# Attention and two MoE layers on one core: the general path as a loop over query tiles, one factor worked out on the row, the last output tiles in another order

## The chip, the cores and the metric

The kernel runs on one core of a Trainium2 chip. The metric is the device time of one execution in microseconds (us). TensorE is called PE here, its weight loads PEld, VectorE DVE, ScalarE ACT, GpSimd POOL and SyncE SP. A letter q behind an engine's name (PEldq, DVEq, SPq) is its sequencer, which runs branches, waits and the issue of DMAs.

## The reference

Local attention with a few global keys and a distance bias, then a layer with SiLU and a layer with hard-swish, in float32.

```python
# q, k, v: (2, 8, 768, 64); n_global = 8, n_local = 96
scores = q @ k.transpose(0, 1, 3, 2) / 8
rel = pos[:, None] - pos[None, :]
keep = (pos[None, :] < n_global) | ((rel >= 0) & (rel < n_local))
dist = where(is_global & ~is_local, n_local, abs(rel))
a = softmax(where(keep, scores - slope[h] * dist, -1e9))
x = (a @ v) as (1536, 512)
h = x @ moe_w_in;   x = (h * sigmoid(h)) @ moe_w_out            # 512 -> 2048 -> 512
h = x @ moe2_w_in;  y = (h * clip(h + 3, 0, 6) / 6) @ moe2_w_out
```

## The kernel before

The program is written by hand: one block of code for each engine, with semaphores between them. `either` (L205) reads a flag that DVE works out from the two counts and branches on every engine: `banded` when at most 32 global keys and at most 97 local ones are asked for, else `general`. With 8 and 96, `banded` runs. In each engine's stream of instructions the code stands in this order: what is ahead of `either`, the banded body, a jump over the general body, the general body, what follows. On PE the jump is written at L209, and the general body that it skips has `2 * 6 * (2 + 6 + 6)` = 168 matmuls of the attention loop and the 42 of one step of `product`, each with its weight load.

The attention has 48 units (8 pairs of heads, 6 query tiles of 128). What follows are 4 blocks of 8 steps: two halves of the tokens through the first layer, two through the second. A step `s` multiplies by 256 columns of `w_in` in the seven products of a Strassen scheme (`product`, P1, P2, P6, P5, P7, P3, P4 in this order, 6 matmuls of 384 columns each), applies the gate, and multiplies by `w_out` (`down`), one step late. Every matmul is done in three float32r passes (`hi*hi`, `hi*lo`, `lo*hi`), so each weight and activation is split: ACT writes the `_hi` copies (`w_high`, `g_high`, `wo_high`), DVE the `_lo` parts (`w_low`, `g_low`), POOL the sums of `w_in` that the scheme needs (`w_sum`, four for each step) and `wo_low`.

The order around the end of the attention is written out by hand. PE finishes the banded body with all products of step 0 and the last `values`, jumps, and begins step 1. There P1 waits for `g_ok` (the last gate product of step 0, DVE L480), P5 for `c_ok` (the first `c_sum` of step 1, DVE L470), and P7 for the second `kept` of the step, which is ACT's copy `u_c`:

```python
elif n == P7:
    pe.wait_ge(kept, 3 * s + 2)
```

ACT's queue has in step 1 `keep(s, p1_c, 0, P1)`, then `w_high(2, 0)`, then `keep(s, u2_c, 0, P6)`. `w_high(2, 0)` waits for the four sums of step 2, which POOL makes in order after `wo_low(0)`, and `wo_low(0)` waits for the same `g_ok`. DVE's queue has `g_low(0, 0)`, `c_sum(1, 0)`, `g_low(0, 1)`, `w_low(2, 0)`.

At the end, PE does the last `down2` tile by tile (6 matmuls of 512 columns each), ACT copies tiles 0, 2 and 4 from PSUM, DVE tiles 1, 3 and, in two halves, 5, and SP stores each.

Of the kernel before, what the change touches and what calls it, by code (L numbers as in the profile page):

```python
# [12 lines left out]
P = 128  # L13
# [8 lines left out]
GLOB = 32  # L22
# [29 lines left out]


def at_least(eng, sem, value):

    if isinstance(value, int) and value <= 0:
        return
    eng.wait_ge(sem, value)


def build(nc, qT, kT, v, w_in1, w_out1, w_in2, w_out2, counts, out):
    outer = ExitStack()
    with outer:
# [18 lines left out]
        words = sb("words", [1, 4], I32)  # L82
        cnt = sb("cnt", [1, 8])
        ones = sb("ones", [1, P])
# [7 lines left out]
        with attn:  # L92
# [19 lines left out]
            with ExitStack() as general:  # L112

                a_tmp = [sb(f"a_tmp{i}", [P, S], F32, general) for i in range(7)]
                a_rel = sb("a_rel", [P, S], F32, general)
                a_far = sb("a_far", [P, S], F32, general)
# [55 lines left out]
        a_max = sem("a_max"); a_exp = sem("a_exp"); a_norm = sem("a_norm"); a_pt = sem("a_pt")  # L172
        a_prt_ok = sem("a_prt_ok"); a_pv = sem("a_pv"); a_x = sem("a_x")

# [42 lines left out]
        def _(sp):  # L217
# [32 lines left out]
            for s in range(2, NSTEP):  # L250
# [6 lines left out]
            for t in range(NT - 1):  # L257
                store(1, t)
            for a in range(2):
                sp.wait_ge(y_dve, HALF * 3 + HALF + a)  # L260
                sp.dma_start(out[1, NT - 1][:, QC * a:QC * a + QC], y_out[:, NT - 1, QC * a:QC * a + QC]).then_inc(stored, 16)
            sp.wait_ge(stored, 16 * (2 * NT + 1))

        @block.gpsimd
        def _(pool):
# [94 lines left out]
            def general():  # L360

                pool.wait_ge(k_in[1], NQK)
                pool.wait_ge(q_in[1], NQK)
                nc.gpsimd.iota(a_rel[:, :], [[-1, S]], base=0, channel_multiplier=1, **io).then_inc(iota_ok, 1)
                nc.gpsimd.iota(a_tmp[1][:, :], [[1, S]], base=0, channel_multiplier=0, **io).then_inc(iota_ok, 1)
# [22 lines left out]
        def _(dve):  # L388
            links = [0]

            def link(ins):

                links[0] += 1
                ins.then_inc(chain, 1)
                dve.wait_ge(chain, links[0])


            for h in range(2 * NH):
# [15 lines left out]
            nc.vector.tensor_scalar(cnt[:, 6:7], cnt[:, 5:6], 0.0, None, ALU.max).then_inc(row_ok, 1)  # L414
            link(nc.vector.tensor_scalar(cnt[:, 7:8], cnt[:, 5:6], 1.0, None, ALU.is_ge))
            link(nc.vector.scalar_tensor_tensor(cnt[:, 7:8], cnt[:, 5:6], float(MAXLOC), cnt[:, 7:8], ALU.is_le, ALU.mult))
            nc.vector.scalar_tensor_tensor(flag[:, :], cnt[:, 4:5], float(GLOB), cnt[:, 7:8], ALU.is_le,
                                           ALU.mult).then_inc(flag_ok, 1)
# [113 lines left out]
            def general():  # L532
                rel, jj, loc, glb, keep, ngl, dist = [a[:, :] for a in a_tmp]
                halves = lambda ap: ap.rearrange("p (a k) -> p a k", a=2)
# [7 lines left out]
                dve.sem_inc(a_score, 1)  # L542
                NLINK = 126

                with dve.Fori(0, NPAIR) as it:
                    count = [0]

                    def link(ins):

                        count[0] += 1  # L550
                        ins.then_inc(a_link, 1)
                        dve.wait_ge(a_link, NLINK * it + count[0] + 1)


                    for t in range(NT):
                        link(nc.vector.tensor_scalar(rel, a_rel[:, :], float(P * t), None, ALU.add))
                        masks(link, rel, jj, loc, glb, keep, ngl, dist)
                        link(nc.vector.tensor_scalar(a_far[:, :], keep, -MASKED, MASKED, ALU.mult, ALU.add))
                        for h in range(2):
# [15 lines left out]
                            nc.vector.tensor_scalar(a_pr[:, :], a_pr[:, :], a_one[:, 4:5], None, ALU.mult).then_inc(a_norm, 1)  # L575

                    assert count[0] == NLINK, count[0]
                for s in range(2):
# [80 lines left out]
            for a in range(2):  # L659
                nc.vector.tensor_copy(y_out[:, NT - 1, QC * a:QC * a + QC], y_bank(NT - 1)[:, QC * a:QC * a + QC]).then_inc(y_dve, 1)  # L660

        @block.scalar
        def _(act):
# [110 lines left out]
            def general():  # L774
                act.sem_inc(a_x, 1)
                with act.Fori(0, NPAIR) as it:
                    for t in range(NT):
                        for h in range(2):
# [7 lines left out]
                        act.wait_ge(a_pv, 2 * NT * it + 2 * t + 2)  # L786
                        nc.scalar.activation(x_raw[:, bass.ds(it, 1), P * t:P * t + P].rearrange("p a t -> p (a t)"),
                                             ps[:, 4, 0:P], ACT.Copy).then_inc(a_x, 1)
# [70 lines left out]
            act.wait_ge(stored, 16 * NT)  # L859
            for t in (0, 2, 4):  # L860
                act.wait_ge(y_tile, t + 1)
                nc.scalar.activation(y_out[:, t, :], y_bank(t), ACT.Copy).then_inc(y_act, 1)

        @block.tensor
        def _(pe):
# [104 lines left out]
            def general():  # L970
                with pe.Fori(0, NPAIR) as it:
                    for t in range(NT):
                        for h in range(2):
                            step = 2 * NT * it + 2 * t + h + 1
                            if t == 0 and h == 0:
                                pe.wait_ge(k_in[0], NQK * (it + 1))
                                pe.wait_ge(q_in[0], NQK * (it + 1))
                                pe.wait_ge(v_in[0], 16 * (it + 1))
                            pe.wait_ge(a_score, step)
                            for b in range(2):  # L980
# [32 lines left out]

            def down2(s, c, t):

                for n, (wo, g) in enumerate(((wo_hi, g_hi), (wo_lo, g_hi), (wo_hi, g_lo))):
                    mm = nc.tensor.matmul(y_bank(t), g[:, s % 2, c, P * t:P * t + P], wo[:, s % 2, DM * c:DM * c + DM],  # L1017
                                          start=s % STEPS == 0 and c == 0 and n == 0,
                                          stop=s % STEPS == STEPS - 1 and c == 1 and n == 2)
                return mm  # L1020
# [35 lines left out]
            pe.wait_ge(g_lo_ok, 2 * s + 2)  # L1056
            for t in range(NT):
                down2(s, 0, t)
                down2(s, 1, t).then_inc(y_tile, 1)

# [44 lines left out]
```

## Time and profile before

| | us |
|---|---|
| median of 3 runs | 605.09 |
| lowest, highest | 604.94, 606.37 |
| profiled execution | 604.28 |
| its span | 602.2 |

| engine | busy us | share of the span |
|---|---|---|
| PE | 591.2 | 98% |
| PEld | 515.6 | 86% |
| DVE | 374.9 | 62% |
| ACT | 341.3 | 57% |
| POOL | 285.1 | 47% |

The span is the time from the first to the last instruction of the core; 2.1 us of the profiled execution's time lie around it. Busy PE counts pipelined matmuls with modelled ends, so 98% means that matmuls follow each other nearly everywhere. What counts is where they don't, and what each of these gaps waits for.

### The profile page before, as it was taken

How to read it: one execution, taken by the hardware profiler on the slowest of the kernel's cores; microseconds unless marked ns; L12 is line 12 of the kernel's file. 1: busy time of each engine (PE TensorE's matmuls, PEld its weight loads, DVE VectorE, ACT ScalarE, POOL GpSimd, SP SyncE). 2: the span in 40 equal slices, each digit the busy share in tenths (PEclk: the TensorE clock that was granted, in tenths of full speed). 3: DMA queues.
4: the chain of work that ended last, by engine and by line, in shares of the span. 5: the costliest groups of instructions: out<-in, count | busy, mean ns of one | idle time of the engine just before them, and what ended most of it. 6: DMA issues, size and time to landing. Idle time of an engine off the chain costs nothing.

```text
span 602.2 us, 9602 instructions
## 1 busy us (share of the span) xinstructions
PE 591.2 (98%) x3423; PEld 515.6 (86%) x3423; DVE 374.9 (62%) x697; ACT 341.3 (57%) x658; POOL 285.1 (47%) x353
## 2 busy tenths in 40 slices
PE   7999998999999999999999999999999999999997
PEld 4665557999999999999999998999999989999996
DVE  6678985766755568557555966575556685555331
ACT  6789886445454467444444665544457565555441
POOL 4787994757933314439433234395333343331110
PEclk9999999899999999999999999999999999999999
DMA  8434430132222112211222123113221252220002
GB/s 355 152 116 169 151 119 4 36 140 72 70 71 71 71 35 89 85 53 56 71 70 71 36 70 106 70 36 101 72 69 41 70 175 70 71 71 35 1 0 106
DMA packets 14597, 50.08 MB, mean 83 GB/s; under 512 B 1618, under 2 KB 1874, under 8 KB 14546
## 3 DMA queue, kind: packets, MB, share of 16 engines
q1 hardware_dynamic: 14258, 48.63, 23.5%
q10 hardware_dynamic: 288, 0.79, 0.4%
q8 instruction: 29, 0.48, 0.3%
q14 instruction: 22, 0.18, 0.1%
HBM read 46.27 MB, written 3.15 MB: 82 GB/s over the span
## 4 chain that ended last, share of the span: by engine, by line
PE 88%; POOL 6%; issue 2%; ACT 2%; DVE 2%; DVEq 0%; DMA 0%; ACTq 0%
PE ps L941 38%; PE ps L1017 22%; PE ps L1008 15%; PE ps L1009 8%; POOL probs L283 3%; PE ps L888 2%; PE ps L898 2%; PE ps L913 2%; POOL rsume L275 1%; ACT probs L673 1%; POOL x_t L323 0%; POOL x_t L320 0%; POOL x_t L315 0%; DVE x_lo L464 0%; DVE g_f L480 0%
## 5 line engine op out<-in xcount | busy, mean ns | idle before, releaser
L328 POOL TENSOR_TENSOR wo_lo<-wo_raw,wo_hi 128x1024 fp32r<-128x1024 f32 x32 | 77.3, 2416 | 258.8 <-ACT wo_hi L741 251.4
L941 PE MATMUL ps<-x_hi,wi_hi 128*128 128x384 f32 x448 | 151.5, 338 | 2.3 <-issue 2.3
L941 PE MATMUL ps<-x_lo,wi_hi 128*128 128x384 f32 x448 | 150.7, 336 | 0.0
L941 PE MATMUL ps<-x_hi,wi_lo 128*128 128x384 f32 x448 | 150.5, 336 | 0.0
L470 DVE TENSOR_TENSOR c_sb<-ps,p_c 128x384 f32<-128x384 f32 x64 | 35.6, 557 | 159.3 <-PE ps L941 159.3
L721 ACT ACTIVATE p_c<-ps 128x384 f32<-128x384 f32 x64 | 31.5, 492 | 126.4 <-PE ps L941 126.0
L941 PEld LDWEIGHTS ps<-x_hi,wi_hi 128*128 128x128 f32 x448 | 84.6, 189 | 5.5 <-issue 2.8
L941 PEld LDWEIGHTS ps<-x_hi,wi_lo 128*128 128x128 f32 x448 | 84.6, 189 | 0.5
L941 PEld LDWEIGHTS ps<-x_lo,wi_hi 128*128 128x128 f32 x448 | 84.6, 189 | 0.0
L1017 PE MATMUL ps<-wo_hi,g_lo 128*128 128x512 f32 x192 | 75.0, 391 | 0.0
L1017 PE MATMUL ps<-wo_lo,g_hi 128*128 128x512 f32 x192 | 75.0, 390 | 0.0
L1017 PE MATMUL ps<-wo_hi,g_hi 128*128 128x512 f32 x192 | 74.7, 389 | 0.0
L809 ACT ACTIVATE g_hi<-g_f 128x768 fp32r<-128x768 f32 x64 | 50.6, 839 | 42.4 <-DVE g_f L480 25.3
L455 DVE TENSOR_TENSOR wi_lo<-wi_raw,wi_hi 128x896 fp32r<-128x896 f32 x64 | 71.9, 1157 | 0.2 <-ACT wi_hi L702 0.2
L702 ACT ACTIVATE wi_hi<-wi_raw 128x896 fp32r<-128x896 f32 x64 | 57.4, 938 | 2.3 <-POOL wi_raw L300 2.3
L1008 PE MATMUL ps<-g_hi,wo_lo 128*128 128x512 f32 x128 | 50.0, 391 | 0.0
L1008 PE MATMUL ps<-g_lo,wo_hi 128*128 128x512 f32 x128 | 50.0, 391 | 0.0
L1008 PE MATMUL ps<-g_hi,wo_hi 128*128 128x512 f32 x128 | 50.0, 391 | 0.0
L673 ACT ACTIVATE probs<-negs,negmax 128x256 f32<-128x256 f32 (+1 forms) x96 | 45.9, 480 | 6.2 <-DVE negmax L491 5.8
L283 POOL TENSOR_SCALAR probs<-probs,rinv 128x256 f32<-128x256 f32 (+1 forms) x96 | 45.2, 484 | 4.1
L491 DVE CUSTOM_DVE_ANT_0 negs<-ps,m_bias 128x256 f32<-128x256 f32 (+1 forms) x96 | 37.3, 391 | 15.8 <-PE ps L888 12.6
L1017 PEld LDWEIGHTS ps<-wo_hi,g_lo 128*128 128x128 f32 x192 | 36.0, 188 | 7.5
(95 smaller groups left out, 1095.1 us busy)
## 6 DMA issues: line engine op xcount, KB each, us to landing
wi_raw<-in_w_in SPq DMA_DIRECT2D x32, 512.0 KB, 3.4
wo_raw<-in_w_out SPq DMA_DIRECT2D x32, 512.0 KB, 3.4
v_raw<-in_v SPq DMA_DIRECT2D x8, 704.0 KB, 4.2
k_raw<-in_kT SPq DMA_DIRECT2D x8, 464.0 KB, 4.9
out_y<-y_out SPq DMA_DIRECT2D x11, 256.0 KB, 4.5
q_raw<-in_qT SPq DMA_DIRECT2D x6, 384.0 KB, 5.8
q_raw<-in_qT ACTq DMA_DIRECT2D x2, 384.0 KB, 4.0
out_y<-y_out SPq DMA_DIRECT2D x2, 128.0 KB, 1.8
```

The source lines that it names most:

```text
L283: nc.gpsimd.tensor_scalar(probs[:, u % DEEP, h, a:256], probs[:, u % DEEP, h, a:256], rinv[:, u % DEEP, h:h + 1], 1.0, ALU.mult, ALU.mult) ...
L328: nc.gpsimd.tensor_tensor(wo_lo[:, s % 2, :], wo_raw[:, s % 2, :], wo_hi[:, s % 2, :], ALU.subtract).then_inc(wo_lo_ok, 1)
L455: nc.vector.tensor_tensor(wi_lo[:, s % 2, at], wi_raw[:, s % 2, QC + 7 * P * part:QC + 7 * P * part + 7 * P], wi_hi[:, s % 2, at], ALU.sub ...
L470: nc.vector.tensor_tensor(c_sb[:, i, :], p_bank(bank), add[:, :], ALU.add).then_inc(c_ok, 1)
L491: nc.vector.tensor_tensor_reduce(negs[:, u % 2, h, 0 if t else P:256], sc, bi, -0.125, 3.0e38, ALU.add, ALU.min, negmax[:, u % DEEP, h:h + ...
L673: nc.scalar.activation(probs[:, u % DEEP, h, a:256], negs[:, u % 2, h, a:256], ACT.Exp, bias=negmax[:, u % DEEP, h:h + 1], scale=-1.0, acc ...
L702: nc.scalar.activation(wi_hi[:, s % 2, at], wi_raw[:, s % 2, QC + 7 * P * part:QC + 7 * P * part + 7 * P], ACT.Copy).then_inc(wi_hi_ok, 1)
L809: nc.scalar.activation(g_hi[:, s % 2, f, :], g_f[:, f, :, :].rearrange("p a t -> p (a t)"), ACT.Copy, scale=1.0 if s < NSTEP // 2 else 1.0 ...
L941: mm = nc.tensor.matmul(p_bank(bank), w[:, s % 2, at], x[:, b, k, :], start=fresh and k == 0 and i == 0, stop=k == 1 and i == 2, skip_grou ...
L1008: nc.tensor.matmul(y_bank(i), wo[:, s % 2, w], g[:, s % 2, c, 0:512], start=first, stop=last)
L1009: mm = nc.tensor.matmul(y_bank(4 + i // 2)[:, 256 * (i % 2):256 * (i % 2) + 256], wo[:, s % 2, w], g[:, s % 2, c, 512:S], start=first and ...
L1017: mm = nc.tensor.matmul(y_bank(t), g[:, s % 2, c, P * t:P * t + P], wo[:, s % 2, DM * c:DM * c + DM], start=s % STEPS == 0 and c == 0 and ...
```

## The change

The general path, which does not run with these inputs, becomes a loop over the query tiles inside the loop over pairs, on PE, DVE and ACT. On the path that runs, DVE works out `-8 * n_local` on the one-row tile `cnt` before the flag, where `base` did it later on 128 partitions; the broadcast matmul carries four columns for three, and waits for two semaphore steps. The last `down2` goes by the table `LAST`: tiles 0 to 3, the first half of tile 4, tile 5, the second half of tile 4.

```diff
+LAST = ((0, 0, slice(0, DM)), (1, 1, slice(0, DM)), (2, 2, slice(0, DM)), (3, 3, slice(0, DM)),
+        (4, 4, slice(0, QC)), (5, 5, slice(0, DM)), (6, 4, slice(QC, DM)))
+LAST_DVE = (1, 3, 6)
...
+            for i, t, cols in LAST:
+                dve_before = sum(j < i for j in LAST_DVE)
+                if i in LAST_DVE:
+                    sp.wait_ge(y_dve, HALF * 3 + dve_before + 1)
+                else:
+                    sp.wait_ge(y_act, HALF * 3 + i - dve_before + 1)
+                sp.dma_start(out[1, t][:, cols], y_out[:, t, cols]).then_inc(stored, 16)
...
             nc.vector.tensor_scalar(cnt[:, 6:7], cnt[:, 5:6], 0.0, None, ALU.max).then_inc(row_ok, 1)
+            nc.vector.tensor_scalar(cnt[:, 7:8], cnt[:, 5:6], -8.0, 0.0, ALU.mult, ALU.min).then_inc(row_ok, 1)
...
-                link(nc.vector.tensor_copy(nums[:, 0:3], ps[:, 1, 0:3]))
+                link(nc.vector.tensor_copy(nums[:, :], ps[:, 1, 0:4]))
...
-                link(nc.vector.tensor_scalar(nums[:, 3:4], nl, -8.0, None, ALU.mult))
...
-            for t in (1, 3):
-                dve.wait_ge(y_tile, t + 1)
-                nc.vector.tensor_copy(y_out[:, t, :], y_bank(t)).then_inc(y_dve, 1)
-            dve.wait_ge(y_tile, NT)
-            for a in range(2):
-                nc.vector.tensor_copy(y_out[:, NT - 1, QC * a:QC * a + QC], y_bank(NT - 1)[:, QC * a:QC * a + QC]).then_inc(y_dve, 1)
+            for i, t, cols in LAST:
+                if i in LAST_DVE:
+                    dve.wait_ge(y_tile, i + 1)
+                    nc.vector.tensor_copy(y_out[:, t, cols], y_bank(t)[:, cols]).then_inc(y_dve, 1)
...
-            pe.wait_ge(row_ok, 1)
-            nc.tensor.matmul(ps[:, 1, 0:3], ones[:, :], cnt[:, 4:7], start=True, stop=True).then_inc(rows_ok, 1)
+            pe.wait_ge(row_ok, 2)
+            nc.tensor.matmul(ps[:, 1, 0:4], ones[:, :], cnt[:, 4:8], start=True, stop=True).then_inc(rows_ok, 1)
...
                 with pe.Fori(0, NPAIR) as it:
-                    for t in range(NT):
+                    with pe.Fori(0, NT) as t:
                         for h in range(2):
...
-                                                      q_raw0[D * h:D * h + D, P * t:P * t + P],
+                                                      a_q[D * h:D * h + D, :],
...
-            for t in range(NT):
-                down2(s, 0, t)
-                down2(s, 1, t).then_inc(y_tile, 1)
+            for i, t, cols in LAST:
+                if cols.start:
+
+                    pe.wait_ge(y_act, HALF * 3 + 3)
+                down2(s, 0, t, cols)
+                down2(s, 1, t, cols).then_inc(y_tile, 1)
```

Three places in the order of instructions. The first is PE, from the last `values` of the banded body through the jump (L209) into the general body; `a_pr` and `a_prT` are that body's probabilities. Before:

```order
L913 MATMUL ps<-probsT,v_raw 64x128 x4
L209 UNCONDITIONAL_BRANCH
L971 UNCONDITIONAL_BRANCH
L971 ISA
L979 ISA
L981 MATMUL ps<-k_raw,q_raw 128x384 x2
L988 MATMUL ps<-ident,a_pr 128x128 x6
L992 ISA
L995 MATMUL ps<-a_prT,v_raw 64x128 x6
L979 REGISTER_ALU
```

and of the change, at the same place:

```order
L926 MATMUL ps<-probsT,v_raw 64x128 x4
L215 UNCONDITIONAL_BRANCH
L984 UNCONDITIONAL_BRANCH
L985 UNCONDITIONAL_BRANCH
L985 ISA
L991 ISA
L993 ISA
L995 MATMUL ps<-k_raw,a_q 128x384 x2
L1002 MATMUL ps<-ident,a_pr 128x128 x6
L1009 MATMUL ps<-a_prT,v_raw 64x128 x6
L991 REGISTER_ALU
```

The group of 2, 6 and 6 matmuls stands 12 times before and twice in the change, 168 and 28 matmuls; the 42 of `product` follow in both. The jump at the head leads past all of it.

The second is DVE ahead of and behind the branch of `either`, up to the first wide operation of `base`. Before:

```order
L414 TENSOR_SCALAR cnt<-cnt 1x1
L415 TENSOR_SCALAR cnt<-cnt 1x1
L416 SCALAR_TENSOR_TENSOR cnt<-cnt 1x1
L417 SCALAR_TENSOR_TENSOR flag<-cnt 1x1
L208 TENSOR_LOAD flag
L208 ISA x2
L209 COMPARE_AND_BRANCH
L424 COPY nums<-ps 128x3
L440 TENSOR_SCALAR nums<-nums 128x1
L442 TENSOR_SCALAR x_t<-x_t,nums 128x384
```

and of the change:

```order
L422 TENSOR_SCALAR cnt<-cnt 1x1
L423 TENSOR_SCALAR cnt<-cnt 1x1
L424 TENSOR_SCALAR cnt<-cnt 1x1
L425 SCALAR_TENSOR_TENSOR cnt<-cnt 1x1
L426 SCALAR_TENSOR_TENSOR flag<-cnt 1x1
L214 TENSOR_LOAD flag
L214 ISA x2
L215 COMPARE_AND_BRANCH
L433 COPY nums<-ps 128x4
L450 TENSOR_SCALAR x_t<-x_t,nums 128x384
```

One operation on a single element is added ahead of the flag, and the one at L440 is gone behind the branch.

The third is SP's queue at the end of the program, the last weights and the stores of the second half of the tokens. Before:

```order
L194 DMA wi_raw<-in_w_in 128x1024
L199 DMA wo_raw<-in_w_out 128x1024 x2
L248 DMA out_y<-y_out 128x512 x5
L261 DMA out_y<-y_out 128x256 x2
L63 UNCONDITIONAL_BRANCH
```

and of the change:

```order
L200 DMA wi_raw<-in_w_in 128x1024
L205 DMA wo_raw<-in_w_out 128x1024 x2
L269 DMA out_y<-y_out 128x512 x4
L269 DMA out_y<-y_out 128x256
L269 DMA out_y<-y_out 128x512
L269 DMA out_y<-y_out 128x256
L68 UNCONDITIONAL_BRANCH
```

A whole tile now stands between the two halves, and the halves are of tile 4.

## Rows read from the trace of the kernel before

**Rows 1.** The page, part 1: busy time of each engine.

```profile
PE 591.2 (98%) x3423; PEld 515.6 (86%) x3423; DVE 374.9 (62%) x697; ACT 341.3 (57%) x658; POOL 285.1 (47%) x353
```

**Rows 2.** The page, part 4: the chain that ended last, by line.

```profile
PE ps L941 38%; PE ps L1017 22%; PE ps L1008 15%; PE ps L1009 8%; POOL probs L283 3%; PE ps L888 2%; PE ps L898 2%; PE ps L913 2%; POOL rsume L275 1%; ACT probs L673 1%; POOL x_t L323 0%; POOL x_t L320 0%; POOL x_t L315 0%; DVE x_lo L464 0%; DVE g_f L480 0%
```

**Rows 3.** Line 209 by engine: count, duration min/median/max in ns, first and last start.

```profile
L209 ACTq COMPARE_BRANCH  x2: 43/44/45, 3.8 to 103.5; - x2
L209 PEldq COMPARE_BRANCH  x2: 78/2039/4000, 3.9 to 101.5; - x2
L209 DVEq COMPARE_BRANCH  x2: 50/56/63, 4.0 to 97.7; - x2
```

**Rows 4.** The same chain in order of time: start us, us, what.

```profile
102.97 1.04 DVE g_f L480 x2
104.01 1.69 issue
105.70 9.16 PE ps L941 x42
114.86 0.23 PE ps L1008
115.09 0.12 PE ps L1009
...
123.19 7.28 PE ps L941 x42
```

**Rows 5.** Stretches: length, busy PE, PEld, DVE, ACT, POOL, granted clock, DMA share, GB/s.

```profile
103.44:105.70 2.26, 0.00 (x1) 0.03 (x1) 1.44 (x3) 2.03 (x3) 1.62 (x1) 1.00 0.01 4
...
106.55:109.97 3.42, 3.42 (x13) 3.42 (x12) 1.45 (x3) 0.49 (x1) 3.34 (x4) 0.50 0.47 153
110.00:114.70 4.70, 4.70 (x28) 4.62 (x27) 3.58 (x5) 3.01 (x6) 4.62 (x6) 1.00 0.00 0
```

**Rows 6.** POOL in order of time after 104 us: start us, us, what [idle before].

```profile
104.08 2.36 POOL L328 TENSOR_TENSOR wo_lo<-wo_raw,wo_hi 128x1024 fp32r<-128x1024 f32 x1 [7.36 <-DVE g_f L480]
106.40 1.45 POOL L292 TENSOR_TENSOR wi_raw<-wi_raw 128x256 f32<-128x256 f32 x1
...
109.30 0.73 POOL L300 TENSOR_TENSOR wi_raw<-wi_raw 128x256 f32<-128x256 f32 x1
109.99 1.46 POOL L292 TENSOR_TENSOR wi_raw<-wi_raw 128x256 f32<-128x256 f32 x1
```

**Rows 7.** ACT in order of time after 107 us.

```profile
107.30 0.49 ACT L721 ACTIVATE p_c<-ps 128x384 f32<-128x384 f32 x1 [1.78 <-PE ps L941]
110.07 0.96 ACT L702 ACTIVATE wi_hi<-wi_raw 128x896 fp32r<-128x896 f32 x1 [2.27 <-POOL wi_raw L300]
110.93 0.47 ACT L721 ACTIVATE u_c<-ps 128x384 f32<-128x384 f32 x1
```

**Rows 8.** DVE in order of time after 104 us.

```profile
104.82 2.44 DVE L598 TENSOR_TENSOR g_lo<-g_f,g_hi 128x768 fp32r<-128x768 f32 x1 [0.82 <-ACT g_hi L809]
109.22 0.56 DVE L470 TENSOR_TENSOR c_sb<-ps,p_c 128x384 f32<-128x384 f32 x1 [1.97 <-PE ps L941]
109.70 1.15 DVE L598 TENSOR_TENSOR g_lo<-g_f,g_hi 128x768 fp32r<-128x768 f32 x1
```

**Rows 9.** PE in order of time: the 25th matmul of step 1, P7's first.

```profile
111.53 0.36 PE L941 MATMUL ps<-x_hi,wi_hi 128*128 128x384 f32 x1
```

**Rows 10.** The chain at the start of the program.

```profile
2.61 0.07 DVE cnt L415
...
4.26 0.16 DVE nums L440
4.43 0.03 issue
```

**Rows 11.** The end: DVE and SP in order of time, and one stretch.

```profile
599.14 0.76 DVE L660 COPY y_out<-ps 128x256 f32<-128x256 f32 x2 [2.03 <-PE ps L1017]
599.59 0.81 SPq L261 DMA_DIRECT2D out_y<-y_out  x2
...
600.40:601.40 1.00, 0.00 (x0) 0.00 (x0) 0.00 (x0) 0.00 (x0) 0.00 (x0) 1.00 0.78 262
```

More of the change, by code:

```diff
@@ L112, in build @@
             with ExitStack() as general:
-                a_tmp = [sb(f"a_tmp{i}", [P, S], F32, general) for i in range(7)]
+                a_tmp = [sb(f"a_tmp{i}", [P, S], F32, general) for i in range(6)]
                 a_rel = sb("a_rel", [P, S], F32, general)
+                a_q = sb("a_q", [P, P], F32, general)
                 a_far = sb("a_far", [P, S], F32, general)
@@ L256, in _ @@
                         store(0, t)
-            for t in range(NT - 1):
-                store(1, t)
-            for a in range(2):
-                sp.wait_ge(y_dve, HALF * 3 + HALF + a)
-                sp.dma_start(out[1, NT - 1][:, QC * a:QC * a + QC], y_out[:, NT - 1, QC * a:QC * a + QC]).then_inc(stored, 16)
-            sp.wait_ge(stored, 16 * (2 * NT + 1))
+            for i, t, cols in LAST:
[5 more added lines that the diff above has]
+                sp.dma_start(out[1, t][:, cols], y_out[:, t, cols]).then_inc(stored, 16)
+            sp.wait_ge(stored, 16 * (NT + len(LAST)))
         @block.gpsimd
@@ L414, in _ @@
             nc.vector.tensor_scalar(cnt[:, 6:7], cnt[:, 5:6], 0.0, None, ALU.max).then_inc(row_ok, 1)
[L415 to L417 removed]
+            nc.vector.tensor_scalar(cnt[:, 7:8], cnt[:, 5:6], -8.0, 0.0, ALU.mult, ALU.min).then_inc(row_ok, 1)
+            link(nc.vector.tensor_scalar(cnt[:, 8:9], cnt[:, 5:6], 1.0, None, ALU.is_ge))
+            link(nc.vector.scalar_tensor_tensor(cnt[:, 8:9], cnt[:, 5:6], float(MAXLOC), cnt[:, 8:9], ALU.is_le, ALU.mult))
+            nc.vector.scalar_tensor_tensor(flag[:, :], cnt[:, 4:5], float(GLOB), cnt[:, 8:9], ALU.is_le,
                                            ALU.mult).then_inc(flag_ok, 1)
@@ L532, in general @@
             def general():
-                rel, jj, loc, glb, keep, ngl, dist = [a[:, :] for a in a_tmp]
+                jj, loc, glb, keep, ngl, dist = [a[:, :] for a in a_tmp]
                 halves = lambda ap: ap.rearrange("p (a k) -> p a k", a=2)
@@ L542, in general, with link @@
                 dve.sem_inc(a_score, 1)
-                NLINK = 126
+                NLINK = 22
                 with dve.Fori(0, NPAIR) as it:
[L546 to L552, printed above, removed]
-                    for t in range(NT):
-                        link(nc.vector.tensor_scalar(rel, a_rel[:, :], float(P * t), None, ALU.add))
-                        masks(link, rel, jj, loc, glb, keep, ngl, dist)
+                    with dve.Fori(0, NT) as t:
+                        count = [0]
+                        def link(ins):
+                            count[0] += 1
+                            ins.then_inc(a_link, 1)
+                            dve.wait_ge(a_link, (NLINK * NT + 1) * it + NLINK * t + count[0] + 1)
+                        masks(link, a_rel[:, :], jj, loc, glb, keep, ngl, dist)
                         link(nc.vector.tensor_scalar(a_far[:, :], keep, -MASKED, MASKED, ALU.mult, ALU.add))
@@ L775, in general @@
                 act.sem_inc(a_x, 1)
+                x_tiles = x_raw[:, :, :].rearrange("p n (t k) -> p (n t) k", k=P)
                 with act.Fori(0, NPAIR) as it:
-                    for t in range(NT):
+                    with act.Fori(0, NT) as t:
+                        act.wait_ge(q_in[0], NQK * (it + 1))
+                        act.wait_ge(a_score, 2 * NT * it + 2 * t + 1)
+                        nc.scalar.activation(a_q[:, :], q_raw0[:, bass.ds(P * t, P)], ACT.Copy).then_inc(a_qt, 1)
                         for h in range(2):
@@ L859, in _ @@
             act.wait_ge(stored, 16 * NT)
-            for t in (0, 2, 4):
-                act.wait_ge(y_tile, t + 1)
-                nc.scalar.activation(y_out[:, t, :], y_bank(t), ACT.Copy).then_inc(y_act, 1)
+            for i, t, cols in LAST:
+                if i not in LAST_DVE:
+                    act.wait_ge(y_tile, i + 1)
+                    nc.scalar.activation(y_out[:, t, cols], y_bank(t)[:, cols], ACT.Copy).then_inc(y_act, 1)
         @block.tensor
@@ L1012, in down1, with down2 @@
                 return mm
-            def down2(s, c, t):
+            def down2(s, c, t, cols=slice(0, DM)):
                 for n, (wo, g) in enumerate(((wo_hi, g_hi), (wo_lo, g_hi), (wo_hi, g_lo))):
-                    mm = nc.tensor.matmul(y_bank(t), g[:, s % 2, c, P * t:P * t + P], wo[:, s % 2, DM * c:DM * c + DM],
-                                          start=s % STEPS == 0 and c == 0 and n == 0,
-                                          stop=s % STEPS == STEPS - 1 and c == 1 and n == 2)
+                    mm = nc.tensor.matmul(y_bank(t)[:, cols], g[:, s % 2, c, P * t:P * t + P],
+                                          wo[:, s % 2, DM * c + cols.start:DM * c + cols.stop], start=s % STEPS == 0 and c == 0 and n == 0,
+                                          stop=s % STEPS == STEPS - 1 and c == 1 and n == 2, skip_group_check=True)
                 return mm
@@ L1056, in _ @@
             pe.wait_ge(g_lo_ok, 2 * s + 2)
-            for t in range(NT):
-                down2(s, 0, t)
-                down2(s, 1, t).then_inc(y_tile, 1)
+            for i, t, cols in LAST:
+                if cols.start:
+                    pe.wait_ge(y_act, HALF * 3 + 3)
+                down2(s, 0, t, cols)
+                down2(s, 1, t, cols).then_inc(y_tile, 1)
 def kernel(q, k, v, n_global, n_local, moe_w_in, moe_w_out, moe2_w_in, moe2_w_out):
```

20 lines of the change are left out of this document (11 added, 9 removed).

## The prediction

> **What bounds the kernel now.** I read the page first. PE is busy in 98% of the span [rows 1], and the chain that ended last lies on PE's matmuls for most of its length [rows 2]. So the time moves by what lies between PE's matmuls, and most of the changed lines (the general path) never run. In order of time the chain shows one gap that no producer explains: DVE's last gate product ends at 104.01, then 1.69 us of "issue", then PE's 42 products of step 1 from 105.70 [rows 4]. The view of line 209 names it. PE's second branch instruction there, the jump past the general body, lasts 4000 ns from 101.5; the same jump takes 43 ns on ACT and 63 on DVE [rows 3]. PE is idle from 103.44 to 105.70, and the granted clock then falls to 0.50 (1.2 of 2.4 GHz) for 3.4 us from 106.55 [rows 5]. Therefore the 42 products take 9.16 us, where the same 42 of a later step take 7.28 [rows 4].
>
> **The jump.** The length of the skipped code is what differs. PE skips 168 + 42 matmuls with their weight loads, 420 instructions and some dozens of waits and register operations; DVE's jump passes 126 linked operations with a wait each and costs nothing. After the change PE skips 28 + 42 matmuls, 140 instructions and their waits, less than DVE does now. I take PE's jump then at DVE's 63 ns, with 4000 ns as the other end. The Trainium skill has a rule for it (Runtime: NRT & Kernel Launch, section Instruction fetch mechanics): a taken branch whose target lies outside the window of two pages of 256 instructions stalls for a fetch; by it PE's jump would miss before and hit after, the same two values.
>
> Without the stall PE's step 1 starts when P1's own wait for `g_ok` is over, at 104.01 plus the 0.05 or so of a handover, 104.08: 1.6 us earlier. The obvious sum is then 1.6 for the gap plus 9.16 - 7.28 = 1.9 for the clock, 3.5 us less. I don't believe it, because of what is due next.
>
> **Where the stall goes.** P7, the fifth product of the step, waits for ACT's `u_c`. ACT does `u_c` behind `w_high(2, 0)`, which has idled 2.27 us for POOL's fourth sum, and starts at 110.07; `u_c` lies from 110.93 to 111.40 [rows 7], and P7's first matmul starts at 111.53 [rows 9]. POOL's own sequence began at 104.08, released by the same DVE product as P1, and runs without a pause through `wo_low(0)` and four sums until 110.03 [rows 6]. Nothing in it depends on PE's jump. P7 can therefore not start before about 111.45, however early PE comes. Without stall and at full clock PE has done P1, P2, P6 and P5 (24 matmuls at 7.28 / 42 = 0.173, 4.2 us) at 108.3; P5 waits for `c_sum(1, 0)`, which waits for DVE's `g_low(0, 0)` until 107.26 [rows 8], so it rather ends at 109.1. PE then stands for 2.4 us or more before P7. The low clock of the present run fell just where there was this slack. So of 3.5 us nothing is left at P7.
>
> **And two costs come with it.** First, POOL and DVE hold each other up. POOL's sum takes 0.73 us alone, and 1.45 and 1.46 in the two places where it meets a `g_low` of DVE [rows 6, 8]; `g_low(0, 0)` itself takes 2.44 beside `wo_low(0)`, against 1.15 of the next one. Now `c_sum(1, 0)` and `g_low(0, 1)` come at 109.22 and 109.70, when the last sum of step 2 is under way, and hurt only a sum of step 3. In the change PE's P2 is done early, `c_sum(1, 0)` follows `g_low(0, 0)` at 107.26, and `g_low(0, 1)` at 107.8, in the middle of the sums of step 2: one of them costs 0.73 more, and `w_high`, `u_c` and P7 shift to about 112.2. Ends: 0, if POOL holds what they share each time, and 0.95, the whole of a `g_low`. The Trainium skill says why (SBUF — State Buffer, section Who interferes with whom): a VectorE operation with two SBUF inputs and a GpSimd operation that reads SBUF exclude each other for a whole instruction, whoever starts first. By that rule `c_sum`, which reads PSUM, does not collide, and the row of 109.22 beside the sum of 109.30 at 0.73 agrees; the delay would be the same 0.73 to 0.95.
>
> Second, the clock. PE idle for 2.26 us brought it down [rows 5]. In the change PE is idle for 0.6 us at 103.5, some 0.7 before P5 and 2.4 to 3.1 before P7, no less in sum and in one piece longer. I expect it to fall again, now after P7 has started or shortly before, where PE has no slack and the chain is matmuls alone. A low spell on the path costs 9.16 - 7.28 = 1.9 us; if it begins in the gap some of it is hidden. I take 1.6, with ends 0 and 1.9.
>
> **The small parts.** Start: the chain passes through L440, 0.19 us with its handover [rows 10], which goes; ahead of the flag one more operation on one element costs the 0.07 of L415 [rows 10], and the branch chain behind the flag shifts by it. Net -0.1; the fourth column of the small matmul is nothing beside these. End: the split of tile 4 replaces 6 matmuls of 0.23 by 12 of 0.12 (the two paces of the chain [rows 4]), +0.1. Behind the last matmul stand two copies, 0.76 us, and two issues [rows 11]; one copy and one issue stay, about -0.35. But tile 5's 256 KB is now issued only about half a us before the last 128 KB, and at the 262 GB/s of the stretch in which the final 256 KB went [rows 11] these two need 1.5 us in the queue, one behind the other. So about half of the gain is lost. End: -0.15, bounds -0.3 and +0.1. The wait for ACT's copy of the first half of tile 4 is covered by the 6 matmuls of tile 5 (1.4 us against a copy below 0.76). ACT's and DVE's own jumps cost nothing now and cannot gain.
>
> **Sum.** Against the profiled execution's 604.28: P7 later +0.7, low clock on the path +1.6, start -0.1, end -0.15, together +2.05, 606.3. The profiled execution is 0.8 below the median of the runs, 605.09; they spread over 1.4 us, and I read this as the low spell falling in other places of the same step, outside the slack that it found in the profiled one. On the median the sum gives 607.1. As the other runs already pay some of the clock, I forecast between the two, **606.8 us**, with 605.9 to 607.9 for this case.
>
> **Rivals.** (1) The gain is real: P7 is not held, because POOL's sums come earlier or `u_c` does. PE would be ahead by 1.6 us and, with a shorter idle, keep its clock: 604.3 - 3.5 - 0.25 = 600.5 to 603 on the side of faster. For it speaks only that the gap is the largest "issue" on the chain; against it ACT's 2.27 us of idle for POOL, and POOL's unbroken sequence. It decides if `u_c` ends before 109.8. 10%. (2) The stall goes, P7 waits, but the clock does not fall on the path (the idle pieces are short enough, or the spell lies in the gap): only the collision is left, 605.09 + 0.7 - 0.25 = 605.5, or 604.8 without it. For it speaks that PE's new idle is cut in three by P1 to P5; against it the 2.26 us in one piece that were enough, and the last piece is as long. 15%. (3) The jump is no cheaper: something other than the length of the skipped code makes PE's 4000 ns, its queue for one. Then only start and end are left, 604.8. The jump of DVE, also long, speaks mildly for it. 12%. The forecast itself has 60%; 3% is for the rest, such as other pieces of code that now lie across a fetch.
>
> **Range and chances.** What a measurement of this kernel can tell from no change is about 0.3%, 1.8 us. The forecast case is nearly half above 606.9, where slower begins, and half below; the rivals (2) and (3) are all within. Slower 0.36 with a little for a late clock in (2), within 0.3% 0.54, faster 0.10, which is rival (1). The range has to take in (2) and (3) and leaves out (1): 604.5 to 607.9.
>
> **What would show it.** In the profile of the changed kernel the branch at L215 on PE lasts under 0.1 us and step 1 starts at about 104 (if 4000 again: rival 3). P7's first matmul starts at 111.4 to 112.4 behind an idle of over 2 us put down to ACT's `u_c` (if at 108 to 110: rival 1). `g_low(0, 1)` starts before 108 and one of the sums of step 2 takes about 1.45. The granted clock is at 0.50 for some 3.4 us within 109 to 116. The last copy is one of 256 columns. The prediction is wrong above all if `u_c` is not what PE waits for next, or if the clock stays up.

## The result, and the profile after

Median of the changed kernel 608.98 us (606.38 to 610.46, 19 runs), of the kernel before on the same chip 606.24 (602.90 to 607.79, 19 runs): ratio 1.0050, 95% interval 1.0036 to 1.0064. It is slower, and 1.1 us above the upper end of the range predicted. The ratios here and below leave out runs in the slow state and are not the quotients of the two medians.

The forecast started from 605.09 us, the median of 3 runs of the kernel before. With 19 runs that median is 606.24, so 1.15 us of the distance to the forecast lie in this base. The change itself was forecast at +0.28% (606.8 for 605.09) and measured at +0.50%.

The profiled execution took 607.72 us, its span is 606.0 against 602.2. Part 1 of the page of the changed kernel answers to [rows 1]: six matmuls more, and PE busy for 3.5 us more.

```profile
PE 594.7 (98%) x3429; PEld 516.4 (85%) x3429; DVE 369.2 (61%) x696; ACT 341.6 (56%) x659; POOL 284.1 (47%) x353
```

Line 215 by engine (count, min/median/max in ns, first and last start) answers to [rows 3]. PE's jump past the general body is 310 ns for 4000:

```profile
L215 PEldq COMPARE_BRANCH  x2: 78/194/310, 4.0 to 100.0; - x2
L215 DVEq COMPARE_BRANCH  x2: 50/56/63, 4.0 to 96.3; - x2
```

The chain in order of time (start us, us, what) answers to [rows 4]. The "issue" of 1.69 is gone from behind the gate product; in its place the chain leaves PE and goes through POOL's four sums and ACT's `u_c` to P7:

```profile
101.50 1.04 DVE g_f L488 x2
102.61 2.40 POOL wo_lo L336
105.01 1.40 POOL wi_raw L300
106.42 1.41 POOL wi_raw L302
107.83 0.69 POOL wi_raw L305
108.58 0.73 POOL wi_raw L308
109.62 0.57 issue
110.20 0.48 ACT u_c L728
110.72 4.76 PE ps L954 x18
```

PE in order of time, the instructions that it idled ahead of (in brackets how long, and for whom): P1 follows at once, P5 waits 0.31, P7 waits 3.05 for ACT.

```profile
102.68 0.41 PE L954 MATMUL ps<-x_hi,wi_hi 128*128 128x384 f32 x1 [0.73 <-DVE g_f L488]
106.35 0.44 PE L954 MATMUL ps<-x_hi,wi_hi 128*128 128x384 f32 x1 [0.31 <-DVE c_sb L478]
110.72 0.69 PE L954 MATMUL ps<-x_hi,wi_hi 128*128 128x384 f32 x1 [3.05 <-ACT u_c L728]
```

Two stretches (start and end, then length, busy PE, PEld, DVE, ACT, POOL, granted clock, DMA share, GB/s) answer to [rows 5]: the idle piece, in which POOL is busy nearly throughout, and the spell at 0.50 that follows it, now partly on PE's own path:

```profile
107.66:110.72 3.06, 0.01 (x1) 0.00 (x1) 0.40 (x1) 1.38 (x3) 2.98 (x6) 0.94 0.02 7
110.32:113.74 3.42, 3.02 (x9) 3.02 (x10) 1.85 (x2) 1.24 (x4) 3.34 (x4) 0.50 0.00 0
```

DVE and POOL in order of time show the collision. `g_low(0, 1)` comes at 106.22, which is 3.7 us after the last gate product; in [rows 8] it is 5.7 us. The second sum of `w_in`, at 106.38, takes 1.44 for the 0.73 that it takes alone in [rows 6]:

```profile
105.75 0.55 DVE L478 TENSOR_TENSOR c_sb<-ps,p_c 128x384 f32<-128x384 f32 x1
106.22 1.02 DVE L607 TENSOR_TENSOR g_lo<-g_f,g_hi 128x768 fp32r<-128x768 f32 x1
106.38 1.44 POOL L302 TENSOR_TENSOR wi_raw<-wi_raw 128x256 f32<-128x256 f32 x1
```

So far it is what was forecast in kind. Counted from the end of the last gate product of step 0, step 2 starts after 21.13 us, in the kernel before after 19.03: +2.1. P7 starts 0.65 us later (8.19 for 7.54), and from there to step 2 it is 1.45 more, at the low clock. The prediction had 0.7 and 1.6 for these two, +2.3.

**Where the rest is.** The two spans differ by 3.8 us. The attention ended 1.5 us earlier in this execution; over the traces of this case the gate product ends anywhere from 102.5 to 105.8, so that is scatter. Step 1 gives +2.1, and from the start of step 2 to the end it is 482.33 us for 479.16, +3.2, where the prediction saw only the end of the program, at -0.15. The chain of the changed kernel shows a step of `down2` in the second layer and the last piece:

```profile
539.33 8.40 PE ps L1031 x36
...
586.43 16.83 PE ps L1031 x78
```

And the chain of the kernel before, for the same:

```profile
567.23 8.20 PE ps L1017 x36
...
582.74 16.38 PE ps L1017 x72
```

The same 36 matmuls take 8.40 for 8.20. One such step as a stretch, first of the changed kernel, then of the kernel before:

```profile
539.17:547.57 8.40, 8.40 (x38) 6.76 (x37) 6.15 (x8) 4.10 (x6) 0.93 (x1) 1.00 0.05 19
```

```profile
536.05:544.26 8.21, 8.21 (x38) 6.77 (x37) 6.16 (x8) 4.11 (x6) 0.94 (x1) 1.00 0.08 32
```

PE doesn't wait in either, the clock is 1.00 in both, and the other engines and the transfers do the same or less. Each `down2` matmul is 5.5 ns slower, 0.2333 us for 0.2278 from start to start (8.40 and 8.20 over 36), in all 16 steps of the second layer, 16 x 0.2 = 3.2 us. The products stay as they were, 7.30 us for 42 in both. A step of `down` in the first layer has 24 pairs, each a matmul of 512 and one of 256 columns; a pair takes 0.3472 for 0.3466, 0.015 us in a step and 0.2 in the layer. With 0.25 gained at the end this makes the +3.2. The diff as shown ahead of the prediction leaves out the one line that touches this:

```diff
-        cnt = sb("cnt", [1, 8])
+        cnt = sb("cnt", [1, 9])
```

SBUF is the memory in which the tiles stand. They are placed there one behind the other in steps of 32 bytes; no trace prints the places, so they are worked out here from the declared shapes. With nine words for eight everything allotted behind `cnt` stands 32 bytes further on. `g_hi` and `g_lo` are behind it, `wo_hi`, `wo_lo`, the `x` and the `wi` tiles ahead of it. A `down2` matmul reads one tile of each kind: it loads `g` as weights and streams `wo`.

### The profile page after: what moved, and what is told of

Read it like the earlier page. It is cut to its first block, busy times and chain, and to the rows that moved or that the text cites. A ratio compares the mean times of both kernels' runs of the same rounds, so it can differ in the third digit from the quotient of the medians.

```text
span 606.0 us, 9614 instructions
## 1 busy us (share of the span) xinstructions
PE 594.7 (98%) x3429; PEld 516.4 (85%) x3429; DVE 369.2 (61%) x696; ACT 341.6 (56%) x659; POOL 284.1 (47%) x353
## 4 chain that ended last, share of the span: by engine, by line
PE 88%; POOL 6%; ACT 2%; DVE 2%; issue 1%; DMA 0%; DVEq 0%; ACTq 0%
PE ps L954 38%; PE ps L1031 22%; PE ps L1022 14%; PE ps L1023 8%; POOL probs L291 3%; PE ps L926 2%; PE ps L911 2%; PE ps L901 2%; POOL rsume L283 1%; ACT probs L680 1%; POOL wo_lo L336 0%; POOL x_t L323 0%; POOL x_t L328 0%; DVE x_lo L472 0%; DVE g_f L488 0%
## 5 line engine op out<-in xcount | busy, mean ns | idle before, releaser
L1031 PE MATMUL ps<-wo_hi,g_lo 128*128 128x512 f32 (+1 forms) x194 | 76.3, 393 | 0.0
L1031 PE MATMUL ps<-wo_lo,g_hi 128*128 128x512 f32 (+1 forms) x194 | 76.3, 393 | 0.0
L1031 PE MATMUL ps<-wo_hi,g_hi 128*128 128x512 f32 (+1 forms) x194 | 76.2, 393 | 0.0
```

Of the source, the lines that this page charges most:

```text
L1031: mm = nc.tensor.matmul(y_bank(t)[:, cols], g[:, s % 2, c, P * t:P * t + P], wo[:, s % 2, DM * c + cols.start:DM * c + cols.stop], start=s ...
```

## The experiments

Theory A: the place of `g_hi` and `g_lo` costs the 3.2 us. Rival B: something in the code of the general path or in step 1 does. A third question is what the jump alone is worth, and a fourth, whether `u_c` is really all that PE waits for. The medians are of 5 to 12 runs, those of the kernel before of 17 to 33; each ratio is to runs of the kernel before on the same chip. The expectations give the old pace as 0.2272 us; over a whole step it is 0.2278.

**e1_before_cnt9**: the kernel before, with that one line.

```diff
-        cnt = sb("cnt", [1, 8])
+        cnt = sb("cnt", [1, 9])
```

> The kernel before with one edit: cnt has 9 words for 8, and every tile allotted behind it (g_hi, g_lo, y_out, the attention's tiles) lies 32 bytes further on. No instruction changes. Theory A (places in memory): the 36 matmuls of a down2 step take 8.39 us for 8.20 as in the changed kernel, 16 steps, so 3.0 us or 0.5% slower than before, with step 1 as before (jump of 4.0 us, P7 at once behind P5). Theory B (the pace of down2 comes from the changed code, or from the chip in that one execution): no difference from before, pace 0.2272 us.

608.49 against 604.98, ratio 1.0066 (1.0041 to 1.0091). From step 2 to the end 482.60, for 479.16. The chain has the slow step:

```profile
569.34 8.40 PE ps L1017 x36
```

One word more on a one-row tile makes the old program 0.4 to 0.9% slower. Its step 1 is also worth a look (PE in order of time): with the long jump the start of P1 is late, and P7 idles all the same.

```profile
103.73 0.41 PE L941 MATMUL ps<-x_hi,wi_hi 128*128 128x384 f32 x1 [1.73 <-issue]
110.76 0.44 PE L941 MATMUL ps<-x_hi,wi_hi 128*128 128x384 f32 x1 [2.59 <-ACT u_c L721]
```

Here the granted clock stays at 1.00, and step 2 starts 19.74 after the gate product; the expectation, that P7 follows P5 at once as in [rows 4], did not come true. The profiled execution of [rows 4] and [rows 5] had the low spell right behind the jump; in this one nothing held P2 back, so `c_sum` and `g_low(0, 1)` came early (106.11 and 106.59) and met the third sum, which took 1.44. The collision is thus no property of the change:

```profile
107.10 1.44 POOL L297 TENSOR_TENSOR wi_raw<-wi_raw 128x256 f32<-128x256 f32 x1
```

**e2_after_aligned**: the changed kernel with `cnt` as `[1, 17]`, which puts the tiles behind it 64 bytes from their old places. If what counts were 64-byte alignment, the pace would be back.

```diff
-        cnt = sb("cnt", [1, 9])
+        cnt = sb("cnt", [1, 17])
```

> The changed kernel with cnt of 17 words, so that all tiles behind it lie 64 bytes further on than before instead of 32. Theory A (places in memory): down2 goes back to 0.2272 us a matmul, about 3 us less than the changed kernel, and what is left against before is the 2.1 us of step 1 less 0.2 of start and end: 0.2 to 0.35% slower than before. Theory B (code or chance): as the changed kernel, 0.5% slower than before.

611.61 against 604.98, 1.0117 (1.0090 to 1.0144): slower still. `down2` keeps its slow pace, and now the first layer is slow too, 0.3528 for a pair (0.15 us more in each of its 16 steps). The chain, then one step of `down` as a stretch in e2 and in the kernel before:

```profile
574.40 8.40 PE ps L1031 x36
```

```profile
132.37:140.84 8.47, 8.47 (x50) 7.39 (x49) 6.57 (x8) 3.96 (x6) 1.31 (x2) 1.00 0.15 51
```

```profile
130.30:138.62 8.32, 8.32 (x49) 7.33 (x49) 7.88 (x7) 3.96 (x6) 6.57 (x5) 1.00 0.19 64
```

Alignment to 64 bytes is refuted; the place as such is not.

**e3_short_general**: the kernel before with the general path of the change alone, in the same tiles; start, `cnt` and the end of the program are the old ones.

```diff
-                    for t in range(NT):
+                    with pe.Fori(0, NT) as t:
...
-                                                      q_raw0[D * h:D * h + D, P * t:P * t + P],
+                                                      a_q[D * h:D * h + D, :],
```

> The kernel before with the general path of the changed one, and nothing else of the change (cnt of 8 words, the broadcast of 3 columns, the old last tiles). Theory A (the short jump moves the stall to P7 and the low clock behind it): PE's jump under 0.4 us, idle of 3 us before P7, 12.5 us for the 42 products of step 1 against 8.8 (first to last start), step 2 starts 2.1 us later counted from DVE's last gate product: 0.2 to 0.4% slower than before. Rival (the 0.5% comes from memory places alone and the step 1 loss is made up later): no difference from before.

606.70 against 604.98, 1.0025 (1.0006 to 1.0043). From step 2 to the end 479.18, the old pace. The jump is 310 ns, and step 1 looks as in the changed kernel, with a longer spell on the path (PE in order of time, then the stretch):

```profile
110.95 0.69 PE L953 MATMUL ps<-x_hi,wi_hi 128*128 128x384 f32 x1 [3.04 <-ACT u_c L728]
```

```profile
109.77:116.60 6.83, 5.65 (x18) 5.65 (x19) 3.26 (x5) 2.97 (x6) 5.74 (x5) 0.50 0.00 0
```

Step 2 starts 22.32 after the gate product, 1.2 later than expected. So B falls for what lies behind step 1, where the code of the general path costs nothing; and the jump that it shortens gives nothing.

**e4_uc_first**: e2's kernel with ACT's `w_high(2, 0)` moved behind the step's last `keep`, so that `u_c` needn't wait for POOL.

```diff
                 keep(s, p1_c, 0, P1)
-                if s == 1:
-                    w_high(2, 0)
...
                 keep(s, p5_c, 1, P5)
+                if s == 1:
+                    w_high(2, 0)
```

> The changed kernel with cnt of 17 words and, in step 1 alone, ACT's u_c and the next p_c ahead of w_high(2, 0). Theory A (P7 waits for u_c only because it is queued behind w_high): P7 follows P5 with at most 0.5 us of idle, the clock stays at 1.00, the 42 products take under 8.0 us, and step 2 starts 3.5 us or so earlier than in the changed kernel: 0.2 to 0.4% faster than before. Rival (another product of POOL or DVE holds P7 or P3 next): the idle of 2 to 3 us comes back at P3, P4 or down, and the time stays at or above that of before.

609.87 against 604.98, 1.0092 (1.0067 to 1.0118), 1.7 us under e2. The traces show 0.63 us of it in step 1; the intervals overlap, and the rest is not told from scatter. P7 starts without idle 4.97 us after the gate product, for 8.19. But two products later, at P4, PE waits again, now for DVE. The clock falls there too, to 0.50 in the microseconds 113 to 115:

```profile
112.42 0.69 PE L954 MATMUL ps<-x_hi,wi_hi 128*128 128x384 f32 x1 [2.42 <-DVE c_sb L478]
```

DVE in order of time shows what stands ahead of that `c_sum` in its queue, `w_low(2, 0)`, which waits for ACT's `w_high`:

```profile
110.59 1.30 DVE L463 TENSOR_TENSOR wi_lo<-wi_raw,wi_hi 128x896 fp32r<-128x896 f32 x1 [3.12 <-ACT wi_hi L709]
```

**e5_both_orders**: e3's kernel, with ACT's order of e4 and DVE's `w_low(2, 0)` behind both later `c_sum`s of the step.

```diff
                 if s == 1:
                     g_low(0, 1)
-                    w_low(2, 0)
...
                 c_sum(s, 2, 1, u2_c, P3)
+                if s == 1:
+                    w_low(2, 0)
```

> e3's kernel (the kernel before with the short general path, its tiles where they were) and, in step 1 alone, two orders changed: ACT's u_c and next p_c ahead of w_high(2, 0), and DVE's w_low(2, 0) behind c_sum(1, 1) and c_sum(1, 2). Theory A (P7 and then P4 wait only for what is queued behind the weights of step 2): no idle of PE over 0.8 us in step 1, clock at 1.00 through it, step 2 starts 16.4 us after DVE's last gate product of step 0 (19.0 before, 22.5 in e3's trace): 2.6 us or 0.4% faster than before. Rival (the gap is the sum of all that POOL has to do for step 2, and comes back in down or at step 2's P1): step 2 starts 18 us or more after that product, same time as before or slower.

602.55 against 606.45, 0.9943 (0.9921 to 0.9965). Step 2 starts 17.67 after the gate product (e3: 22.32; expected 16.4). PE in order of time has only short waits, the longest for the late `w_low`:

```profile
107.91 0.44 PE L954 MATMUL ps<-x_hi,wi_hi 128*128 128x384 f32 x1 [0.31 <-DVE c_sb L476]
121.76 0.44 PE L954 MATMUL ps<-x_hi,wi_hi 128*128 128x384 f32 x1 [1.08 <-DVE wi_lo L461]
```

and the clock stays up where it was at 0.50 in e3:

```profile
108.00:112.00 4.00, 4.00 (x23) 4.00 (x24) 1.98 (x4) 1.68 (x4) 3.92 (x5) 1.00 0.28 110
```

**e6_g_32, e7_g_128, e11_g_256, e8_all_32**: the kernel before with nothing but a tile of padding, 32, 128 or 256 bytes, ahead of `g_hi`; and with 32 bytes ahead of `x_raw`, which moves both operands of each matmul together.

```diff
+        sb("g_pad", [P, 8])            # e6; [P, 32] in e7, [P, 64] in e11
         g_hi = sb("g_hi", [P, 2, 2, 2 * TB], F32R)
```

```diff
+        sb("x_pad", [P, 8])            # e8
         x_raw = sb("x_raw", [P, NPAIR, S])
```

> The kernel before with 32 bytes left free ahead of g_hi: only g_hi, g_lo and y_out lie 32 bytes further on, everything else is where it was. Theory A (it is g's place, the weights of down2): down2 at 0.2332 us a matmul for 0.2272, down1 at 0.347, the products at 0.1735, 0.5% slower than before. Rival (it is another tile's place, of those that DVE, ACT and POOL work on): down2 stays at 0.2272.

> The kernel before with 128 bytes left free ahead of g_hi, so that g_hi and g_lo start at a multiple of 512 bytes (their 128-column blocks are 512 bytes long). Theory A1 (what counts is where a block of weights begins by itself, and whole 512 bytes are best): down2 at or under 0.2272 us. Theory A2 (what counts is the distance from wo's tiles, which is 0 mod 256 before and not now): down2 at 0.233 or above, down1 pairs at 0.353 as with a shift of 64.

> The kernel before with 32 bytes left free ahead of x_raw: all large tiles lie 32 bytes further on, their distances are as before. Theory A2 (distance between the two tiles that a matmul reads): all paces as before, 0.2272 and 0.1735, time the same. Theory A1 (the place itself): down2 at 0.233 and the products, whose weights move too, above 0.1735 as well; at 6 ns a matmul for all 2500 or so, over 10 us or 2% slower.

> The kernel before with 256 bytes left free ahead of g_hi. If what counts is the distance between the two tiles of a matmul modulo 256 bytes, down2 is at 0.2272 us and a down1 pair at 0.3466, time as before. If it is modulo 512 bytes or more, down2 is at 0.232 or above as with 32, 64 and 128.

| kernel | median, before | ratio (95%) | step 2 to end | 36 matmuls of `down2` |
|---|---|---|---|---|
| e6, g +32 | 608.42, 606.45 | 1.0029 (1.0008 to 1.0051) | 482.61 | 8.40 |
| e7, g +128 | 610.78, 606.45 | 1.0087 (1.0056 to 1.0117) | 483.65 | 8.37 |
| e11, g +256 | 605.16, 606.68 | 0.9983 (0.9959 to 1.0008) | 479.22 | 8.20 |
| e8, all +32 | 604.78, 606.45 | 0.9984 (0.9961 to 1.0006) | 479.20 | 8.20 |

The rows of the chain, of e6, e7, e8 and e11:

```profile
572.56 8.40 PE ps L1018 x36
```

```profile
572.35 8.37 PE ps L1018 x36
```

```profile
569.70 8.20 PE ps L1018 x36
```

```profile
568.74 8.20 PE ps L1018 x36
```

`g_hi` alone by 32 bytes is enough; all tiles together by 32 do nothing. What counts is where `g` stands relative to the tiles ahead of it. The candidate is the distance between the two tiles that a `down2` matmul reads, `g` and `wo`: no other pair is read together by the matmuls that slow down, and the products, which read neither, keep their pace. No run moved `wo` alone, so that it is this pair is argued and not shown. From the declared shapes `g_hi` - `wo_hi` is 63744 bytes, 249 x 256, in the kernel before. 256 more keeps the pace, 32, 64 and 128 more lose it. e7 refutes that any multiple of 128 will do.

These four also have the long jump, and their step 1 shows how it varies with it: P7 idles for over 2 us in e6, e7 and e8, its start is 8.17 to 8.18 after the gate product, and step 2 starts after 19.75, 21.39, 21.44 and, in e11, 19.03. PE's jump is itself not always as long; of line 210, e7 and e11:

```profile
L210 PEldq COMPARE_BRANCH  x2: 87/1704/3320, 3.9 to 100.3; - x2
L210 PEldq COMPARE_BRANCH  x2: 78/1939/3800, 3.9 to 103.0; - x2
```

Of the six traces with the long jump, the two with the longest (4.0 us in the kernel before, 3.8 in e11) have PE idle for 2.26 and 2.10 us ahead of P1, a low spell right behind it, no wait at P7 and the earliest step 2, 19.03. In the other four the jump takes 3.3 to 3.6, PE idles 1.59 to 1.81 ahead of P1, the clock stays up there, and P7 waits. In e7 and e8 the clock fell behind P7's idle, on the path (e8, PE in order of time, and a stretch):

```profile
112.19 0.45 PE L942 MATMUL ps<-x_hi,wi_hi 128*128 128x384 f32 x1 [2.54 <-ACT u_c L722]
```

```profile
113.18:116.60 3.42, 3.42 (x12) 3.42 (x12) 1.54 (x3) 0.91 (x2) 3.34 (x3) 0.50 0.00 0
```

**e9_after_cnt_ahead**: the changed kernel, with `cnt` allotted ahead of `x_raw` and 32 bytes left in its old place, so that every distance is the old one.

```diff
+        cnt = sb("cnt", [1, 9])
         x_raw = sb("x_raw", [P, NPAIR, S])
...
-        cnt = sb("cnt", [1, 9])
+        sb("cnt_pad", [1, 8])
```

> The changed kernel with cnt allotted ahead of x_raw and its old 32 bytes left free, so that all large tiles stand at the distances that they had before; no instruction differs. Theory A (of the 0.5%, half is the place of g, half the low clock that now always follows the idle before P7): down2 at 0.2272 us, 3.2 us less behind step 2's start than the changed kernel (479.0 from there to the end for 482.3), 0.1 to 0.35% slower than before. Rival (the rest of the change costs something of its own): over 0.45% slower.

605.99 against 606.68, 0.9996 (0.9972 to 1.0020), for an expected 1.001 to 1.0035. No loss is left that this interval could tell from none, with every instruction of the change in place, and from step 2 to the end it is 478.92. The chain has the old pace, and shows what the split of tile 4 costs, 16.47 for 16.38:

```profile
568.83 8.20 PE ps L1032 x36
...
584.34 16.47 PE ps L1032 x78
```

**e10_after_cnt_ahead_orders**: e9 with the two moves of e5.

> e9's kernel with the two orders of e5. Against e5 it has the changed start and the changed last tiles too. Theory A: step 1 as in e5 (step 2 starts 17.7 us after the last gate product of step 0), the end 0.1 to 0.3 us shorter than e5's: 0.5 to 0.7% faster than before. Rival (the last tiles cost, by 12 short matmuls and stores that queue): as e5 or 0.1% slower.

602.16 against 606.68, 0.9934 (0.9913 to 0.9954): faster than both kernels. Step 2 starts after 17.68, and the granted clock is 1.00 throughout the 20 us around step 1:

```profile
104.00:124.00 20.00, 18.60 (x106) 17.02 (x105) 16.32 (x16) 9.92 (x17) 12.31 (x11) 1.00 0.21 74
```

**e12_g_low_late**: e3 with DVE's `g_low(0, 1)` behind `w_low(2, 0)`, out of the way of POOL's sums.

```diff
                 if s == 1:
-                    g_low(0, 1)
                     w_low(2, 0)
+                    g_low(0, 1)
```

> e3's kernel with one order changed: in step 1 DVE does g_low(0, 1) behind w_low(2, 0) instead of ahead of it. Theory A (g_low(0, 1) stops one of POOL's sums for 0.7 us, and P7 with it): the second sum takes 0.73 us for 1.44, u_c and P7 come 0.7 us earlier, P7 7.45 us after the last gate product for 8.19. Rival (POOL is slowed by something else, or u_c waits for another): P7 stays at 8.19.

605.49 against 606.68, 0.9999 (0.9977 to 1.0021). The same sum takes 0.73 (POOL in order of time), and P7 starts after 7.48 for 8.19, its idle 2.34 for 3.04:

```profile
107.20 0.73 POOL L300 TENSOR_TENSOR wi_raw<-wi_raw 128x256 f32<-128x256 f32 x1
```

The collision is worth 0.71 us at P7. The clock fell at 111.6 all the same, and step 2 starts after 20.64.

## Why the prediction was wrong

**What held.** The jump was long because of the code that it passes, and shortening the code made it short (rival 3 is false). It is 310 ns and not 63, but that is hidden: P1 starts 0.15 after the gate product. P7 then waits for `u_c`, 3.05 us (rival 1 is false). `g_low(0, 1)` starts before 108 and doubles a sum; e12 gives that 0.71 us. The clock goes to 0.50 for 3.4 us within 109 to 116, partly on the path (against rival 2). All but the length of the branch, which was to be under 0.1 us, is as named ahead, with P7's start counted from the gate product, since the attention ended 1.5 us earlier. Step 1 comes out at +2.1 for the predicted +2.3 against the trace of before. That the stall is worth nothing by itself is shown by e3, and where it went by e4 and e5: behind it stood two more waits, `u_c` in ACT's queue and `c_sum` in DVE's. With one of them moved step 2 starts 0.63 us earlier (20.77 in e4, 21.40 in e2), with both 4.65 us (17.67 in e5, 22.32 in e3).

**The step that failed** is in "the small parts": "the fourth column of the small matmul is nothing beside these". The column is nothing, but the word that it needs lengthens `cnt` and moves the `g` tiles 32 bytes against `wo`. That costs 5.5 ns in each `down2` matmul of 512 columns, 3.2 us in the second layer and 0.2 in the first, together 3.4 us or 0.56%. It was put at 0 with no bound, since I priced instructions, and this edit has none; a list of what stands where in SBUF, or the line of the diff read for itself, would have shown it. No row of the trace of before could have given the price. e1 (the word alone, +0.66%) and e6 (the 32 bytes alone, +0.29%) show the cause; both traces have 3.4 us more between step 2 and the end, which is a little above e6's interval (to 0.51%) and within e1's (0.41 to 0.91%). e9 (all but the shift, 0.9996) shows that nothing else of the change is needed for the loss.

**Two terms were off in size.** The end: from the start of the last step of `down2` to the end of the program it is 19.36 us in e9 for 19.61 in the kernel before, and 19.72 in the changed kernel for 20.04 in e1, which has the same slow pace. So the end gives 0.25 to 0.3 us, where I had 0.15 with 0.3 as the bound. The split costs the predicted 0.1 (16.47 for 16.38), which is already taken off. The copies and stores of the changed kernel show it: DVE's last copy is done 0.5 us after SP's issues of the last two stores began, so the last store is queued close behind that of tile 5, as I had assumed. The gain is larger than forecast, which says that the two lose less to each other than the 262 GB/s of [rows 11] let me expect; no run took it apart.

```profile
602.57 0.60 ACT L875 ACTIVATE y_out<-ps 128x512 f32<-128x512 f32 x1 [1.01 <-PE ps L1031]
603.19 0.87 SPq L269 DMA_DIRECT2D out_y<-y_out  x2
603.28 0.42 DVE L667 COPY y_out<-ps 128x256 f32<-128x256 f32 x1 [2.13 <-PE ps L1031]
```

And step 1: +2.3 is near the +2.1 of the one profiled execution, but that was a favourable one. With the long jump the traces give 19.03 to 21.44 us to the start of step 2 (six of them, on average 20.1, with the low spell on the path in two). With the short one they give 20.64 to 22.32 (five, e12 with its one order among them, on average 21.4, with a spell in each). The difference of these averages, 1.3 us, is the estimate that the traces allow. The measured worth of the short jump alone is a loss, 1.0025 (1.0006 to 1.0043) in e3, and e9, which has it with the cheaper start and end, is at 0.9996 (0.9972 to 1.0020). I had taken the collision and the spell as costs of the change; e1, e6, e7 and e8 have the collision with the long jump too. Without the shift the kernel is at no measurable difference (e9, 605.99 on its chip), where the forecast was +0.28%, above e9's interval. So the forecast was also too high for the terms that it did price, and that it came within 2.2 us is luck: this error and the missing 3.4 us partly cancel, and the low base of 605.09 adds 1.15.

**Left open.** Why PE's pace depends on the place of `g` is not settled, nor that `wo` is the other half of the distance; only 0, 32, 64, 128 and 256 bytes more were tried. Nor is it shown why 64 and 128 slow the first layer (0.3528 and 0.3509 for a pair) where 32 hardly does (0.3472). And how much of the 0 to 0.4% of the short jump is the clock, which falls in another place in each execution, these runs cannot separate. Nor is it shown why the jump takes 3.3 us in one kernel and 4.0 in another, with the same code to pass.

## What to carry to other kernels

Before pricing instructions, check whether a change moves tiles: any tile that grows, however small, shifts what is allotted behind it, and long runs of matmuls can feel it (here by the place of one operand against the tiles ahead of it); put small tiles where they shift both operands or neither, and compare the time of a fixed count of matmuls before and after. A stall on the chain is worth only what the next wait leaves: follow the queues of the engines that feed the next products, and move what stands in them ahead of what PE needs. And look at more than one execution before taking a stretch with a throttled clock as typical.

## What the runs showed of the hardware

The pace of a `down2` matmul depends on how far `g` stands behind the tiles ahead of it. It is 0.2278 us for 512 columns at both of the distances tried that are multiples of 256 bytes from `wo`, and 0.2333 at 32 bytes more, with no wait and the clock at 1.00. Moving all tiles by 32 bytes changes nothing (8.20 for 36 in e8). PE's taken branch cost 3.3 to 4.0 us past the general body with its 210 matmuls and 0.31 past one with 70, where DVE's, past 126 operations, is 0.06. A sum of POOL that takes 0.73 us alone took 1.44 beside DVE's `g_low`, and 0.73 again with `g_low` moved away (e12). The granted clock fell to 0.50 within or behind idle pieces of 2.1 to 3.1 us in ten traces, but not around 2.59 and 2.72 us ahead of P7 in e1 and e6, and not in e5 and e10, where no piece at step 1 is longer than 1.1 us.
